# One-hot rows per token tile, one f32 product for the gate weights, and routing tables in two parts, in an attention + MoE + gated-FFN kernel

## What is computed

```python
attn_out = _attn_ref(...)                      # 4 x 8 heads, 576 positions, bias from a small MLP
x = attn_out.transpose(0, 2, 1, 3).reshape(2304, 512)
# _moe_ref: top-1 routing over 8 experts
logits = x @ w_gate                            # 2304 x 8
expert_idx = np.argmax(logits, axis=1)
probs = softmax(logits); gate_w = probs[np.arange(N), expert_idx]
for e in range(8):
    mask = expert_idx == e
    out[mask] = gate_w[mask, None] * (relu(x[mask] @ w1[e]) @ w2[e])     # F = 1024
# _moe2_ref: RMS norm, then (silu(xn @ w_gate) * (xn @ w_val)) @ w_out   # d_ff = 1536
```

## Time and profile before

| | us |
|---|---|
| median of 3 runs | 1083.43 (1083.37 to 1083.89) |
| the profiled execution, whole | 1085.24 |
| its span | 1083.4 |
| of the span, TensorE busy | 1045.8 (97%) |
| VectorE, ScalarE, GpSimd busy | 739.9, 475.5, 203.0 |

### The profile page before, as it was taken

The page is one execution under the profiler, slowest core; times in us unless marked ns, Lnnn a source line. Parts: engine busy times, 40 slices in busy tenths (PEclk is TensorE's granted clock), DMA queues, the critical chain, the costliest instruction groups (busy, mean ns, idle before and its releaser), DMA issues.

```text
span 1083.4 us, 23065 instructions
## 1 busy us (share of the span) xinstructions
PE 1045.8 (97%) x7160; PEld 936.8 (86%) x7161; DVE 739.9 (68%) x1249; ACT 475.5 (44%) x972; POOL 203.0 (19%) x196
## 2 busy tenths in 40 slices
PE   5889999999999899999999999999999999999996
PEld 2368888888887799999999989899999999999995
DVE  8975656656565737757464499877777777677674
ACT  6987777777772525635343342311212212112111
POOL 2036544435330411222121000010100100100101
PEclk9999999999999899999999999999999999999998
DMA  4974654756411845763532350200100100000000
GB/s 132 290 234 102 186 115 110 194 116 185 110 44 37 307 157 122 188 153 108 149 90 68 93 204 1 49 32 0 48 10 0 58 0 29 29 0 0 30 1 30
DMA packets 87126, 103.11 MB, mean 95 GB/s; under 512 B 49536, under 2 KB 60800, under 8 KB 87088
## 3 DMA queue, kind: packets, MB, share of 16 engines
q1 hardware_dynamic: 83056, 89.27, 29.7%
q0 software_dynamic: 4032, 13.37, 4.4%
HBM read 77.25 MB, written 25.37 MB: 95 GB/s over the span
## 4 chain that ended last, share of the span: by engine, by line
PE 85%; DVE 4%; DMA 1%; issue 1%; ACT 1%; POOL 1%; SPq 0%; DVEq 0%; ACTq 0%; POOLq 0%
PE psum L1724 26%; PE psum L1740 13%; PE psum L1240 10%; PE psum L1249 10%; PE psum L563 8%; PE psum L446 7%; PE psum L546 7%; PE psum L576 2%; DVE f_eg L1679 1%; PE psum L1226 1%; DMA f_vraw<-fv 1%; PE psum L1285 0%; DMA e_xin<-x_tokens,e_col 0%; PE psum L876 0%; DVE f_eg L1681 0%
## 5 line engine op out<-in xcount | busy, mean ns | idle before, releaser
L1679 DVE RECIPROCAL f_eg<-f_eg 128x384 f32<-128x384 f32 x72 | 183.4, 2547 | 0.0
L1646 ACT ACTIVATE f_eg<-psum 128x384 f32<-128x384 f32 x72 | 35.4, 492 | 330.7 <-PE psum L1724 330.7
L611 DVE CUSTOM_DVE_ANT_0 a_sc<-psum,a_bias 128x576 f32<-128x576 f32 x144 | 105.4, 756 | 67.8 <-PE psum L446 64.0
L1724 PE MATMUL psum<-f_x,f_ghi 128*128 (+1 forms) x576 | 147.8, 337 | 2.6 <-DVE f_eg L1683 1.4
L1724 PE MATMUL psum<-f_x,f_vhi 128*128 (+1 forms) x576 | 146.1, 334 | 0.0
L674 ACT ACTIVATE a_pr<-a_sc,a_nmax 128x576 f32<-128x576 f32 x144 | 111.3, 773 | 26.2 <-DVE a_nmax L611 23.7
L1724 PEld LDWEIGHTS psum<-f_x,f_ghi 128*128 128x128 f32 x576 | 105.6, 188 | 9.5 <-issue 2.9
L1614 POOL DMA_INDIRECT out<-f_ob,f_cols x18 | 17.5, 974 | 466.3 <-ACT f_ob L1632 463.0
L1724 PEld LDWEIGHTS psum<-f_x,f_vhi 128*128 128x128 f32 x576 | 104.0, 188 | 0.0
L446 PE MATMUL psum<-a_khi,a_qs 128*128 128x288 f32 x320 | 96.5, 322 | 1.2 <-DVE a_nmax L611 1.2
L1724 PE MATMUL psum<-f_x,f_glo 128*128 (+1 forms) x288 | 97.1, 337 | 0.0
(11 more groups left out here) (240 smaller groups left out, 2355.2 us busy)
## 6 DMA issues: line engine op xcount, KB each, us to landing
e_raw<-ew SPq DMA_DIRECT2D x16, 1024.0 KB, 10.5
bias_ihj<-b_res SPq DMA_DIRECT2D x36, 288.0 KB, 2.8
a_qraw<-q SPq DMA_DIRECT2D x32, 288.0 KB, 5.2
a_kraw<-k SPq DMA_DIRECT2D x32, 288.0 KB, 5.8
a_bias<-bias_ihj SPq DMA_DIRECT2D x16, 576.0 KB, 7.0
xn_t<-e_yn SPq DMA_DIRECT2D x8, 576.0 KB
a_v<-v SPq DMA_DIRECT2D x32, 128.0 KB, 2.4
x_tokens<-a_xp SPq DMA_DIRECT2D x64, 64.0 KB, 1.7
```

Of the source, the lines that this page charges most:

```text
L611: e.tensor_tensor_reduce(sc[:, h, :].rearrange("p (a s) -> p a s", a=2), s_ps[:, h, :, 0:HALF], bias[:, 2 * s + h, :].rearrange("p (c s) - ...
L1646: e.activation(self.eg[:, k % 2, :], self.g_ps[k % 2][:, 0:CHUNK], ACT.Exp, scale=-1.0).then_inc(self.s_e, 1)
L1679: e.reciprocal(x, x).then_inc(self.s_c, 1)
L1724: mm = e.matmul(acc[:, 0:CHUNK], a, b, start=(q == 0 and i == 0), stop=(q == KD - 1 and i == 2))
```

## The change

The change has six parts.

1. VectorE makes `r_inbt` and `r_inq` tile by tile. Each is a `tensor_scalar` with per-partition scalars (18 of 128 x 48 and 18 of 128 x 128), where two whole-array operations of 128 x 864 and three of 128 x 768 stood.
2. The index product takes each tile as it comes, with one idle matmul between two tiles; the 36 idle matmuls ahead of it stay.
3. The gate product is one f32 product of 48 columns a tile, where an fp32r product of 96 columns stood. `r_inbg` comes from 18 `tensor_scalar` operations of 128 x 48 in place of two of 128 x 864, and the split of the gate weights and the addition of the two halves fall away.
4. The tables come in two parts. Number of blocks, number of runs and the run of each block come first (columns 96 to 127). The rest (columns 0 to 95) is written by `second_tables`, behind the first block's `x_lo`. SyncE, ScalarE and VectorE wait for both parts (`all_tables`), TensorE and GpSimd for the first.
5. The first three gathers read `r_idx` directly, without the copies to `e_col`.
6. The idle matmuls behind the two products are 6 and 6 in place of 9 and 5, and each of the first two transposed subtiles has 3 fill matmuls behind it. Quarter 0 of the low weights moves behind the first part of the tables.

```diff
 # RoutingStage.tensor
         self.idle(e, 36)
         for t in range(NT):
-            if t % 6 == 0:
-                e.wait_ge(self.s_q, sem.at(self.s_q, t // 6 + 1))
+            e.wait_ge(self.s_q, sem.at(self.s_q, 2 * t + 2))
             mm = e.matmul(banks.y[:, 2, 0:NCOL], self.inq[:, t, :], self.inbt[:, t, :], start=(t == 0), stop=(t == NT - 1))
+            if t < NT - 1:
+                self.idle(e, 1)
         mm.then_inc(self.s_i, 1)
-        self.idle(e, 9)
-        e.wait_ge(self.s_g, sem.at(self.s_g, 2))
+        self.idle(e, 6)
         for t in range(NT):
-            mm = e.matmul(banks.y[:, 3, 0:2 * NCOL], self.inq[:, t, :], self.inbg[:, t, :], start=(t == 0), stop=(t == NT - 1))
+            e.wait_ge(self.s_g, sem.at(self.s_g, t + 1))
+            mm = e.matmul(banks.y[:, 3, 0:NCOL], self.inq[:, t, :].bitcast(f32), self.inbg[:, t, :],
+                          start=(t == 0), stop=(t == NT - 1))
         mm.then_inc(self.s_gi, 1)
-        self.idle(e, 5)
+        self.idle(e, 6)
...
 # RoutingStage.vector
-        tt(self.inb[:, :, :], rt.col[:, 0:NCOL].unsqueeze(1).to_broadcast([P, NT, NCOL]), over_c(db[:, :]), ALU.is_equal)
-        tt(self.inbt[:, :, :], self.inb[:, :, :], over_c(rt.tok[:, :]), ALU.mult)
-        for a in range(0, NT, 6):
-            e.tensor_tensor(self.inq[:, a:a + 6, :], rt.col[:, :].unsqueeze(1).to_broadcast([P, 6, P]),
-                            self.dq[:, a:a + 6].unsqueeze(2).to_broadcast([P, 6, P]), ALU.is_equal).then_inc(self.s_q, 1)
+        e.wait_ge(s_v, sem.at(s_v, n[0]))
+        for t in range(NT):
+            e.tensor_scalar(self.inbt[:, t, :], rt.col[:, 0:NCOL], db[:, t:t + 1], rt.tok[:, t:t + 1],
+                            ALU.is_equal, ALU.mult).then_inc(self.s_q, 1)
+            e.tensor_scalar(self.inq[:, t, :], rt.col[:, :], self.dq[:, t:t + 1], None, ALU.is_equal).then_inc(self.s_q, 1)
...
-        for i, g in enumerate((self.gate_hi[:, :].bitcast(f32), self.gate_lo[:, :])):
-            e.tensor_tensor(self.inbg[:, :, NCOL * i:NCOL * i + NCOL], self.inb[:, :, :], over_c(g), ALU.mult).then_inc(self.s_g, 1)
-        self.ew.lo(e, 0, 0, self.ew.lead(0))
+        for t in range(NT):
+            e.tensor_scalar(self.inbg[:, t, :], rt.col[:, 0:NCOL], db[:, t:t + 1], gate[:, t:t + 1],
+                            ALU.is_equal, ALU.mult).then_inc(self.s_g, 1)
...
+        e.wait_ge(self.s_gi, sem.at(self.s_gi, 1))
+        e.tensor_copy(rt.gs[:, :], n_ps[:, 3, 0:NCOL]).then_inc(rt.s_gs, 1)
+        go(e.tensor_copy(tabf[:, 96:96 + NBLK], run[:, 0:NBLK]))
+        go(e.tensor_copy(tabf[:, 112:113], run[:, NBLK:NB]))
+        do(e.tensor_copy(tabf[:, 113:114], inc[:, E:E + 1]))
+        e.tensor_copy(rt.tabs[:, 96:128], tabf[:, 96:128]).then_inc(rt.s_tab, 1)
+        self.ew.lo(e, 0, 0, self.ew.lead(0))
...
 # ExpertStage.gpsimd
         for s in range(NSUB):
-            gather(0, s)
+            e.indirect_dma_start(self.xin[:, s, :], None, self.xd,
+                                 bass.IndirectOffsetOnAxis(ap=rt.idx[:, s:s + 1], axis=0)).then_inc(self.s_in[s], 16)
...
 # ExpertStage.tensor
         for s in range(NSUB):
             turn(0, s)
-        fill(5)
+            fill((3, 3, 5)[s])
...
 # ExpertStage.vector
-        used = self.used(e)
-
         def first_lo(c):
             ew.lo(e, 0, c, ew.lead(c))
         for s in range(NSUB):
             x_lo(0, 0, s)
+        second_tables(e)
+        used = self.used(e)
+        self.all_tables(e)
         first_lo(1)
```

More of the change, by code:

```diff
@@ L835, in __init__ @@
         sb = arena.run(arena.XPAR)
+        self.thr, self.delta = sb("r_thr", [P, NBLK + 1]), sb("r_delta", [P, E])
+        self.owner, self.begin, self.begun, self.here, self.from_run = (
+            sb("r_" + n, [P, NBLK + 1]) for n in ("owner", "begin", "begun", "here", "from_run"))
+        self.run = sb("r_run", [P, NBLK + 1])
+        self.of_run = sb("r_of_run", [P, E, NBLK + 1])
+        self.mine = sb("r_mine", [P, NBLK + 1, E])
+        self.tabf, self.fresh = sb("r_tabf", [P, 128]), sb("r_fresh", [P, NBLK + 1])
         self.lt = sb("r_lt", [P, B, E])
@@ L1011, in vector, with second_tables, go, do @@
         do(e.tensor_tensor_scan(run[:, :], rt.ones[:, 0:NB], begin[:, :], -1.0, ALU.mult, ALU.add))
-        go(e.tensor_copy(tabf[:, 32:32 + NBLK], run[:, 0:NBLK]))
-        go(e.tensor_copy(tabf[:, 17:18], run[:, NBLK:NB]))
-        go(e.tensor_copy(tabf[:, 18:19], inc[:, E:E + 1]))
+        e.wait_ge(self.s_gi, sem.at(self.s_gi, 1))
[5 more added lines that the diff above has]
+        self.ew.lo(e, 0, 0, self.ew.lead(0))
+        self.steps = n[0]
+    def second_tables(self, e):
+        sem, rt, s_v, NB = self.sem, self.rt, self.s_v, NBLK + 1
+        owner, begin, run, tabf, inc = self.owner, self.begin, self.run, self.tabf, rt.inc
+        n = [self.steps]
+        def go(ins):
+            n[0] += 1
+            ins.then_inc(s_v, 1)
+        def do(ins):
+            go(ins)
+            e.wait_ge(s_v, sem.at(s_v, n[0]))
+        def tt(o, a, b, op):
+            do(e.tensor_tensor(o, a, b, op))
         go(e.tensor_tensor(self.mine[:, :, :], owner[:, :].unsqueeze(2).to_broadcast([P, NB, E]),
@@ L1021, in vector @@
                            rt.col[:, 0:E].unsqueeze(2).to_broadcast([P, E, NB]), ALU.is_equal))
-        e.wait_ge(self.s_gi, sem.at(self.s_gi, 1))
-        do(e.tensor_copy(self.gs_hi[:, :], n_ps[:, 3, 0:NCOL]))
-        e.tensor_tensor(rt.gs[:, :], n_ps[:, 3, NCOL:2 * NCOL], self.gs_hi[:, :], ALU.add).then_inc(rt.s_gs, 1)
         tt(self.mine[:, :, :], self.mine[:, :, :], self.delta[:, :].unsqueeze(1).to_broadcast([P, NB, E]), ALU.mult)
@@ L1105, in used, with all_tables @@
         e.wait_ge(self.rt.s_tab, self.sem.at(self.rt.s_tab, 1))
[L1106 removed]
+        return e.value_load(self.rt.tabs[0:1, 113:114], min_val=N // BT, max_val=NBLK)
+    def all_tables(self, e):
+        e.wait_ge(self.rt.s_tab, self.sem.at(self.rt.s_tab, 2))
     def runs(self, e):
[L1109 removed]
+        return e.value_load(self.rt.tabs[0:1, 112:113], min_val=1, max_val=E)
     def run(self, e, i):
[L1112 removed]
+        return e.value_load(self.rt.tabs[0:1, bass.ds(i + 96, 1)], min_val=0, max_val=E - 1)
     def code(self, e, i):
@@ L1188, in gather @@
         def gather(i, s):
-            rows, at = ROWS[s], i % (NBLK + 1) * NSUB + s
-            e.tensor_copy(self.col[:, s:s + 1], rt.idx[:, at:at + 1] if isinstance(i, int) else rt.idx[:, bass.ds(at, 1)])\
-                .then_inc(self.s_col, 1)
-            e.wait_ge(self.s_col, sem.at(self.s_col, i * NSUB + s + 1))
+            rows = ROWS[s]
+            e.tensor_copy(self.col[:, s:s + 1], rt.idx[:, bass.ds(i % (NBLK + 1) * NSUB + s, 1)]).then_inc(self.s_col, 1)
+            e.wait_ge(self.s_col, sem.at(self.s_col, (i - 1) * NSUB + s + 1))
             sem.apart(e, i)
@@ L1810, in _ @@
             route.vector(e)
-            ffn.vector(e, experts.vector(e, ffn.early_lo))
+            ffn.vector(e, experts.vector(e, ffn.early_lo, route.second_tables))
         @blk.gpsimd
```

32 lines of the change are left out of this document (10 added, 22 removed).

## The result

The kernel with the change took 1087.23 us (median of 8 runs, 1086.32 to 1091.79), the kernel before 1083.59 us on the same chip (8 runs, 1083.05 to 1084.64). The ratio is 1.0037 [1.0024, 1.005]: slower by 3.6 us, where 1083.8 was forecast. The profiled execution took 1087.89 us, with a span of 1086.1.

A forecast was written before the change was run, and what follows sets the result against it. TensorE, busy for 97% of the span, was taken as the bound; VectorE's table work would start the first block's third slice 0.4 us later, so 1083.43 plus 0.4 gave 1083.8 us, range 1082.0 to 1086.0.

The forecast's parts named there:

- The place of `x_lo`: End of the routing stage, ahead of the block loop: the last `x_lo` was to end at 371.0 us.
- the 0.47 that TensorE allows: Index product: VectorE keeps up with TensorE if a pair of one-hot operations takes at most 0.47 us.
- the hole and the half clock of the earlier trace: Routing stage: TensorE's 2.05 us wait for the first scaling and 1.2 GHz from 367 to 373 us would go.
- Then comes quarter 1: VectorE behind `x_lo`: 2.4 us of tables, 2.2 of low weights, 0.45 of `hlo`, putting the third slice at 376.05.
- a rival with a chance of 0.12: VectorE slower than reckoned, through table register reads or narrow operations: 0.5 to 2 us more, 1084.3 to 1085.8; chance 0.12.
- The base: First block's third slice: its start at 375.68 us in the kernel before, against which 376.05 gave 0.4 us later.
- Behind that, nothing else is late.: After the first `hlo`: no further loss, with quarter 2 up to 0.4 us later and nothing changed outside the routing stage.
- The clock: TensorE's new wait before the third slice: the clock falls again, +3.7 us, 1087.1; chance 0.10.
- The cover of the index product: 17 idle matmuls among 18 products, 5.93 us: index about 3 us later, won back by the gathers.
- The bound of within 0.2%: Whole kernel: 2.2 us either way, 1081.3 to 1085.6, hardly to be told from no change.
- 0.82 for "same": Whole kernel: chance 0.82 of a time within 0.2%, against 0.13 for slower and 0.05 for faster.

The follow-up runs named there:

- read_ahead: Changed kernel with VectorE's register read of the first table part moved ahead of the second tables; 1087.36 us, ratio 1.0027 to the kernel before.
- tables_early: Changed kernel with the second tables written ahead of the first block's `x_lo` instead of behind it; 1084.81 us, ratio 1.0012 to the kernel before.
- fill_the_wait: Changed kernel with eight fill matmuls in the first block ahead of the third slice; 1086.65 us, ratio 1.0026 to the kernel before.
- whole_onehot: Changed kernel with the old whole-array one-hot matrices and no idle matmuls between the index products; 1085.99 us, ratio 1.0022 to the kernel before.
- before_padded: Kernel before with 76 extra semaphore increments starting TensorE's program and 46 on VectorE ahead of the routing; 1092.16 us, ratio 1.0075 to the kernel before.

## Why the prediction was wrong

The place of `x_lo` was right, though some steps ahead of it were off and made up for each other. The pairs of one-hot operations took 0.41 us (350.05 to 357.03 from the first to the last `r_inq`, over 17), inside the 0.47 that TensorE allows. The gate product took 4.12 us for 4.1. The index came 2.45 us later for 3.0, the third gather 0.3 us later where 0.7 us earlier was forecast (it stands 3.96 us behind the cast, for 2.4), the hole and the half clock of the earlier trace rows went, and `e_xlo` ended 28.5 us behind `r_part` for a forecast of 28.3.

**The step that failed is "Then comes quarter 1".** The sum let quarter 1 start at the cast's end. In the trace 0.80 us lies between, in which VectorE reads the tables into registers. The prediction had this as a rival with a chance of 0.12 and named 0.3 us there as what would show it wrong. The sum's other terms of this step held: 2.4 us of table operations took 2.38 (368.90 to 371.28). So the third slice began 34.3 to 34.4 us behind `r_part`, where 33.4 was forecast; TensorE waited 2.10 us and not 1.6. In read_ahead the gap is gone from its place; in tables_early, with the tables ahead of `x_lo` and the read still behind it, quarter 1 follows `e_xlo` at once, and 2.4 us of the median are back.

This step accounts for 0.9 of the 3.4 us by which the forecast was short (1087.2 for 1083.8). The sum had two other terms wrong:

- *The base.* The +0.4 was taken against 33.0 us behind `r_part` (375.68) in a trace with 6.83 us at half clock. The second trace of before has 31.91. Against it the third slice is 2.5 us later, against the first 1.3.
- *"Behind that, nothing else is late."* At the first `e_y` the two pairs of traces agree on 2.9 and 2.6 us. From there to the FFN the five traces with narrow one-hots take 219.61 to 221.61 us (mean 220.47), the nine others 219.01 to 219.90 (mean 219.33). That is another 1.1 us for which the sum had nothing, and its cause stays open (below).

**What the step missed besides** is that ScalarE was held by the tables too, since it now waits for both parts: its first `e_hhi` started at 372.32, 1.0 us after the cast, though the first slice's 12 matmuls, started at 369.25, were done near 370.9. In this order it cost nothing, as VectorE was later still.

**The clock** fell behind the new wait in one trace of two. The fall that did come was 3.4 us, below the 3.5 at half clock from which the prediction let this rival decide. It costs 1.5 us where it happens: from the third slice to the first `e_y` the first trace of after takes 25.44 us, the second 23.95. Its share in the median isn't resolved; fill_the_wait's median is 0.5 lower.

**The cover of the index product was priced at zero.** The forecast let the gathers win back what the index lost, so that the part cost nothing. Put against the kernel before, that held in the trace. But direct gathers and an early `r_gs` then had nothing to bring: with whole one-hots in the same kernel it is 2.4 to 2.9 us faster at a kept clock. The parts, from runs of the changed kernels at a kept clock, in us: narrow one-hots with idle matmuls between and tables behind `x_lo` +4.8 to +5.3 together (2.4 to 2.9 and 1.9 alone); all the rest -1.7 (1081.4 against the 1083.1 of before on the same chip, at its own clock of 0.994). That these come to about the measured difference is no test, since both are taken from the same runs. The f32 gate product, 4.12 us for 2.21, and the shorter idle runs are in "all the rest" and were never undone alone.

**The bound of within 0.2%** was missed too. The baseline's runs reached from 1081.3 to 1087.4 us over all chips, and whether the clock is kept splits the runs of one kernel by some 5 us, so 0.82 for "same" was too sure of a trace of one execution.

**Open.** What the 1.1 us between the first `e_y` and the FFN are is not shown. Waits of ScalarE for TensorE's products don't set them apart: between 410 and 440 us the longest is 3.8 and 3.7 us in the two traces of after, and 3.7 in that of before. A slow instruction fetch near 420 us (3.2 to 4.2 us) stands in the traces of all five runs with the narrow one-hots and of no other, so it is a rival for that 1.1 us and for part of what whole_onehot won at a kept clock. Against it, tables_early has one of 4.0 us and a stretch of only 219.61; and the kernel before has one of 3.6 us near 694. Whether such fetches cost anything wasn't settled.

## What to carry to other kernels

When work moves behind the last producer of a pipeline, ask what the engine's queue holds between the moved work and the next operation on the path: here a register read, which no busy time shows, came on top of 2.4 us of small operations. A whole-array operation cut into tiles helps only if its consumer was waiting for the first tile. Here the consumer started 0.7 us earlier (11.68 us behind `r_part` for 12.36), but the 36 narrow operations took 7.5 us (349.83 to 357.31) where the five large ones take 4.9 in before_padded's trace (359.20 to 364.08), and the idle matmuls put in to fill the product made it last 6.0 us for 2.6. TensorE never waited for a tile in it. Undo the parts of a composite change one by one and then together: its sum hid losses of about 5 us and a gain of about 2.

## What the hardware showed beside that

- A narrow VectorE `tensor_scalar` comes every 0.205 us, whether it has 48 columns and two per-partition scalars or 128 columns and one, and every 0.22 us in the run of 18 for `r_inbg` (4.01 us). So 128 columns with one scalar cost no more here than 48 with two.
- Reading the tables into registers held VectorE for 0.79 to 0.80 us behind the cast, in two kernels.
- A gather straight from the index took 2.02 or 1.65 us on GpSimd while VectorE ran large operations, 1.20 for the first one beside the narrow ones, and 0.94 to 0.97 otherwise.
- Semaphore increments with nothing to do delayed TensorE's first matmul by 62 ns each, and took 81 ns each on VectorE's queue.
- One wait of 0.45 us ahead of narrow fp32r products was followed by 13.65 us at 1.2 GHz in two traces, and in six runs of ten of the one kernel and two of ten of the other the mean clock was 0.993 or less. With the old order it was followed by 3.4 us in two traces and by nothing in five; with idle matmuls between the products it held at 1.00 in all five traces.
